# Expert stage of a fused attention, MoE and gated-MLP kernel: half of the middle activations transposed by VectorE from PSUM to PSUM

## What is computed

```python
for e in range(E):                      # E = 8
    for k in range(2):
        mask = top2[:, k] == e
        if not mask.any():
            continue
        h = np.maximum(x[mask] @ w1[e], 0.0)            # 384 -> 1024
        out[mask] += top2_w[mask, k, None] * (h @ w2[e])  # 1024 -> 384
```

## Time and profile before

| | |
|---|---|
| median of three runs | 1359.45 us |
| the profiled execution, own time | 1352.85 us |
| its span, first to last instruction | 1351.1 us |
| mean granted TensorE clock | 0.981 |
| TensorE matmul busy | 1259.0 us, 93% |
| VectorE busy | 613.1 us, 45% |
| ScalarE busy | 463.4 us, 34% |
| GpSimd busy | 444.2 us, 33% |
| expert stage, first `hidden` to last output | 327.4 to 854.9 us |

### The profile page before, as it was taken

How to read it: one execution, slowest core, us unless ns; L and a number is a source line. 1 busy time by engine, 2 the same in 40 slices (tenths; PEclk the granted TensorE clock), 3 DMA queues, 4 the chain that set the end, 5 groups by cost and what they waited for, 6 DMA issues and landing times.

```text
span 1351.1 us, 26279 instructions
## 1 busy us (share of the span) xinstructions
PE 1259.0 (93%) x9117; PEld 1164.4 (86%) x9118; DVE 613.1 (45%) x1150; ACT 463.4 (34%) x975; POOL 444.2 (33%) x375
## 2 busy tenths in 40 slices
PE   4999999993999999999999999299999999999998
PEld 3787878772999999999999999299999999999997
DVE  6888888855222222222222222344444444444433
ACT  3555656642222222222222222232323323232321
POOL 8567787734541505050517600320101101010000
PEclk9999999996999999999999999799999999999999
DMA  8223433115313222222222320220101101010000
GB/s 301 74 93 134 127 128 117 58 62 212 133 48 128 75 100 80 97 90 88 100 78 107 116 105 30 59 59 0 54 18 36 48 6 53 18 35 17 0 18 18
DMA packets 36172, 105.43 MB, mean 78 GB/s; under 512 B 4992, under 2 KB 20352, under 8 KB 33664
## 3 DMA queue, kind: packets, MB, share of 16 engines
q1 hardware_dynamic: 26928, 55.62, 12.3%
q0 software_dynamic: 8592, 47.98, 9.9%
q10 hardware_dynamic: 576, 0.79, 0.2%
HBM read 77.83 MB, written 26.54 MB: 77 GB/s over the span
## 4 chain that ended last, share of the span: by engine, by line
PE 76%; POOL 9%; DVE 5%; ACT 4%; issue 4%; DMA 1%; DVEq 0%; SPq 0%; ACTq 0%; POOLq 0%
PE pD L1504 17%; PE pD L1569 10%; PE pA L1569 10%; PE pS L1528 9%; PE pA L1528 8%; PE pA L1582 6%; PE pA L1320 4%; PE pA L1515 4%; PE pS L1582 3%; PE pX L1486 1%; POOL fT L517 1%; POOL prods L552 1%; POOL qk L536 1%; DVE W L961 1%; POOL qk L535 1%
## 5 line engine op out<-in xcount | busy, mean ns | idle before, releaser
L1504 PE MATMUL pD<-we,xsH 128*128 x660 | 210.0, 400 | 0.8 <-issue 0.8
L686 POOL DMA_INDIRECT pair<-y_sorted,y_row x48 | 49.6, 1034 | 369.1 <-DVE z L1240 277.0
L1320 PE MATMUL pA<-W 64*128 64x128 f32 x1920 | 140.4, 287 | 15.8 <-DVE W L961 12.2
L1320 PEld LDWEIGHTS pA<-W 64*128 64x128 f32 x1920 | 118.6, 190 | 34.4 <-DVE W L961 18.3
L1261 DVE TENSOR_TENSOR gs<-pD,sig 128x384 f32<-128x384 f32 x96 | 53.5, 557 | 195.5 <-ACT sig L897 195.3
L1504 PEld LDWEIGHTS pD<-we,xsH 128*128 128x128 f32 x660 | 120.7, 190 | 23.9 <-issue 1.4
L1504 PE MATMUL pD<-we,xsL 128*128 x330 | 129.8, 393 | 0.0
L640 POOL CAST we<-stage 128x3072 fp32r<-128x3072 f32 x14 | 38.5, 2753 | 251.9 <-PE pS L1528 128.5
L855 ACT CAST hidH<-pA 128x512 fp32r<-128x512 f32 x110 | 59.2, 589 | 173.6 <-PE pA L1515 173.6
L897 ACT ACTIVATE sig<-pD 128x384 f32<-128x384 f32 x96 | 47.3, 492 | 206.9 <-PE pA L1569 206.4
L1528 PE MATMUL pS<-we,hidH 128*128 x448 | 116.5, 341 | 1.8 <-issue 1.8
(11 more groups left out here) (200 smaller groups left out, 2747.4 us busy)
## 6 DMA issues: line engine op xcount, KB each, us to landing
stage<-w POOLq DMA_DIRECT2D x14, 1536.0 KB, 9.2
qk<-qk_t SPq DMA_DIRECT2D x24, 512.0 KB, 3.6
xs<-x_sorted SPq DMA_DIRECT2D x55, 192.0 KB, 2.4
y_sorted<-yo SPq DMA_DIRECT2D x55, 192.0 KB, 1.9
fT<-f_t SPq DMA_DIRECT2D x12, 512.0 KB, 4.2
vN<-v_n SPq DMA_DIRECT2D x24, 256.0 KB, 2.7
out<-fin SPq DMA_DIRECT2D x8, 576.0 KB, 2.8
stage<-w SPq DMA_DIRECT2D x2, 1536.0 KB, 13.6
```

The lines of the kernel that those rows point to most:

```text
L686: pool.indirect_dma_start(out=pair[:, j, k], out_offset=None, in_=y_sorted[:, :], in_offset=bass.IndirectOffsetOnAxis(ap=y_row[:, t * TS + ...
L1320: ins = pe.matmul(pA[par][:, s, c * P:(c + 1) * P], both[r, 1, c], both[r, 0, c], start=True, stop=True)
L1504: ins = pe.matmul(pD[:, h * 512:(h + 1) * 512], (xsL if a else xsH)[t.par][:, k * P:(k + 1) * P], we[:, bass.ds(at + (b * WE + k * F + h * ...
```

## The change

For each tile the middle activations are now treated by halves in two different ways. The first half goes as before: ReLU on ScalarE into `hid`, which now holds 512 values (`HF = F // 2`), then four transposes on TensorE. The second half is not rectified first. VectorE transposes it from its PSUM bank (`hidden_bank(t, 1)`, bank 1 of `pD` for even tiles, bank 1 of `pA[1]` for odd ones) into bank 1 of `pA[0]`, by 16 instructions on 32 partitions, each of four 32x32 blocks. It does eight of them before `low_x` and eight after. A new semaphore, `s_ht`, counts them. `high_h` and `low_h` then apply the ReLU to both halves: `high_h` is an ACTIVATE with Relu, `low_h` a `scalar_tensor_tensor` with max and subtract.

The order changes too: TensorE does `turn_hidden(t+1)` ahead of `output(t)`, and `output` waits for each half of `hidL` on its own. ScalarE does `rectify(t+1)` ahead of `high_x(t+2)`, and it takes over `take_y`, at the end of its slot. In the table, column 0 of `more_than` is set to 1 once at the start, so that an expert without rows has one tile. The diff, without the declarations of `HF`, of the semaphore and of the smaller `hid`:

```diff
@@ -368,6 +370,10 @@
         def y_bank(t):
 
             return pS[:, 0:DM] if t.par == 0 else pA[1][:, 0, 0:DM]
+
+        def hidden_bank(t, h):
+
+            return pA[1][:, 1] if h and t.par else pD[:, h * HF:(h + 1) * HF]
 
         def out_bank(j):
 
@@ -841,30 +847,37 @@
 
             def rectify(t):
                 if t.c >= 1:
-                    act.wait_ge(s_th, t.times(2))
-                for k in range(2):
-                    act.wait_ge(s_g1, t.times(2, k + 1))
-                    act.activation(hid[:, k * 512:(k + 1) * 512], pD[:, k * 512:(k + 1) * 512],
-                                   ACT.Relu).then_inc(s_relu, 1)
-
-            def high_h(t):
+                    act.wait_ge(s_th, t.times(1))
+                act.wait_ge(s_g1, t.times(2, 1))
+                act.activation(hid[:], hidden_bank(t, 0), ACT.Relu).then_inc(s_relu, 1)
+
+            def high_h(t, h):
                 if t.c >= 2:
                     act.wait_ge(s_g2, t.times(1))
-                for k in range(2):
-                    act.wait_ge(s_th, t.times(2, k + 1))
-                    act.copy(hidH[t.par][:, k * 512:(k + 1) * 512], pA[0][:, k]).then_inc(s_hh, 1)
+                act.wait_ge(s_ht if h else s_th, t.times(1, 1))
+                act.activation(hidH[t.par][:, h * HF:(h + 1) * HF], pA[0][:, h], ACT.Relu).then_inc(s_hh, 1)
+
+            def take_y(t):
+                act.wait_ge(s_g2, t.times(1, 2))
+                if t.c >= 2:
+                    act.wait_ge(s_ys[t.par], t.over(2, 16))
+                act.copy(yo[t.par][:], y_bank(t)).then_inc(s_yo, 1)
 
             high_x(Tile(0))
             high_x(Tile(1))
             rectify(Tile(0))
-            high_h(Tile(0))
+            for h in range(2):
+                high_h(Tile(0), h)
 
             def slot(t):
+                if (t + 1).before(SLOTS):
+                    rectify(t + 1)
                 if (t + 2).before(SLOTS):
                     high_x(t + 2)
                 if (t + 1).before(SLOTS):
-                    rectify(t + 1)
-                    high_h(t + 1)
+                    for h in range(2):
+                        high_h(t + 1, h)
+                take_y(t)
             slots(act, slot)
 
 
@@ -1072,8 +1085,8 @@
 
             for t in (*aT, *stateB, hits, zero):
                 dve.memset(t[:], 0.0)
-            for t in (ones, ones_row):
-                ins = dve.memset(t[:], 1.0)
+            for t in (ones[:], ones_row[:], more_than[:, :, 0:1]):
+                ins = dve.memset(t, 1.0)
             ins.then_inc(s_clear, 1)
             dve.wait_ge(s_const, 2)
             dve.tensor_reduce(chunk_sum[:], ident[:].rearrange("p (c e) -> p e c", c=HP)[:, 0:2 * E], AX.X,
@@ -1145,8 +1158,8 @@
             dve.tensor_tensor(count[:], pS[:, 0:E], region_row[:, 0], ALU.subtract)
             step(dve.tensor_tensor(count_i[:], pS[0:1, 0:E], region_row[0:1, 0], ALU.subtract))
 
-            step(dve.tensor_tensor(more_than[:], count[:].unsqueeze(2).to_broadcast([P, E, NT]),
-                                   iota_t[:].unsqueeze(1).to_broadcast([P, E, NT]), ALU.is_gt))
+            step(dve.tensor_tensor(more_than[:, :, 1:], count[:].unsqueeze(2).to_broadcast([P, E, NT - 1]),
+                                   iota_t[:, 1:].unsqueeze(1).to_broadcast([P, E, NT - 1]), ALU.is_gt))
             step(dve.tensor_reduce(tiles_of[:], more_than[:], AX.X, ALU.add))
             step(dve.tensor_tensor_scan(ends[:], ones_row[:], tiles_of[:], 0.0, ALU.mult, ALU.add))
             step(dve.tensor_scalar(last[:], ends[0:1, E - 1:E], -1.0, None, ALU.add))
@@ -1181,18 +1194,23 @@
                 dve.tensor_tensor(xsL[t.par][:], pX[:, 0:DM], xsH[t.par][:].bitcast(F32),
                                   ALU.subtract).then_inc(s_xl, 1)
 
-            def low_h(t):
-                for k in range(2):
-                    dve.wait_ge(s_hh, t.times(2, k + 1))
-                    c = slice(k * 512, (k + 1) * 512)
-                    dve.tensor_tensor(hidL[t.par][:, c], pA[0][:, k], hidH[t.par][:, c].bitcast(F32),
-                                      ALU.subtract).then_inc(s_hl, 1)
-
-            def take_y(t):
-                dve.wait_ge(s_g2, t.times(1, 2))
-                if t.c >= 2:
-                    dve.wait_ge(s_ys[t.par], t.over(2, 16))
-                dve.tensor_copy(yo[t.par][:], y_bank(t)).then_inc(s_yo, 1)
+            def turn_hidden(t, tokens):
+                dve.wait_ge(s_g1, t.times(2, 2))
+                if t.c >= 1:
+                    dve.wait_ge(s_hl, t.times(2))
+                by_32 = [b.rearrange("p (c q a) -> p c q a", q=4, a=32) for b in (hidden_bank(t, 1), pA[0][:, 1])]
+                for i in tokens:
+                    for q in range(4):
+                        ins = dve.transpose(by_32[1][32 * q:32 * (q + 1), :, i], by_32[0][32 * i:32 * (i + 1), :, q])
+                if tokens[-1] == 3:
+                    ins.then_inc(s_ht, 1)
+
+            def low_h(t, h):
+                dve.wait_ge(s_hh, t.times(2, h + 1))
+                c = slice(h * HF, (h + 1) * HF)
+                dve.scalar_tensor_tensor(out=hidL[t.par][:, c], in0=pA[0][:, h], scalar=0.0,
+                                         in1=hidH[t.par][:, c].bitcast(F32), op0=ALU.max,
+                                         op1=ALU.subtract).then_inc(s_hl, 1)
 
             low_x(Tile(0))
             low_x(Tile(1))
@@ -1211,14 +1229,19 @@
                               ALU.add).then_inc(s_yrow, 1)
             dve.wait_ge(s_yrow, 3)
             dve.tensor_tensor(y_row[:], row_of[:], shift[:], ALU.add).then_inc(s_yrow, 1)
-            low_h(Tile(0))
+            turn_hidden(Tile(0), (0, 1, 2, 3))
+            for h in range(2):
+                low_h(Tile(0), h)
 
             def slot(t):
+                if (t + 1).before(SLOTS):
+                    turn_hidden(t + 1, (0, 1))
                 if (t + 2).before(SLOTS):
                     low_x(t + 2)
-                take_y(t)
                 if (t + 1).before(SLOTS):
-                    low_h(t + 1)
+                    turn_hidden(t + 1, (2, 3))
+                    for h in range(2):
+                        low_h(t + 1, h)
             slots(dve, slot)
 
 
@@ -1497,33 +1520,35 @@
                 pe.wait_ge(s_we, ready + 1)
                 pe.wait_ge(s_xl, t.times(1, 1))
                 for h in range(2):
-                    if t.c >= 1:
-                        pe.wait_ge(s_relu, t.times(2, h - 1))
+                    if h == 0 and t.c >= 1:
+                        pe.wait_ge(s_relu, t.times(1))
+                    if h == 1 and t.c >= 2:
+                        pe.wait_ge(s_ht, t.times(1, -1))
                     for k in range(KC):
                         for n, (a, b) in enumerate(PARTS):
-                            ins = pe.matmul(pD[:, h * 512:(h + 1) * 512], (xsL if a else xsH)[t.par][:, k * P:(k + 1) * P],
-                                            we[:, bass.ds(at + (b * WE + k * F + h * 512), 512)],
+                            ins = pe.matmul(hidden_bank(t, h), (xsL if a else xsH)[t.par][:, k * P:(k + 1) * P],
+                                            we[:, bass.ds(at + (b * WE + k * F + h * HF), HF)],
                                             start=k + n == 0, stop=k == KC - 1 and n == 2)
                     ins.then_inc(s_g1, 1)
 
             def turn_hidden(t):
-                for h in range(2):
-                    pe.wait_ge(s_relu, t.times(2, h + 1))
-                    if t.c >= 1:
-                        pe.wait_ge(s_hl, t.times(2, h - 1))
-                    for k in range(4):
-                        ins = pe.transpose(pA[0][:, h, k * P:(k + 1) * P], hid[:, (4 * h + k) * P:(4 * h + k + 1) * P],
-                                           ident[:])
-                    ins.then_inc(s_th, 1)
+                pe.wait_ge(s_relu, t.times(1, 1))
+                if t.c >= 1:
+                    pe.wait_ge(s_hl, t.times(2, -1))
+                for k in range(FC // 2):
+                    c = slice(k * P, (k + 1) * P)
+                    ins = pe.transpose(pA[0][:, 0, c], hid[:, c], ident[:])
+                ins.then_inc(s_th, 1)
 
             def output(t):
 
                 at, ready = weights_of(t)
                 pe.wait_ge(s_we, ready + 2)
-                pe.wait_ge(s_hl, t.times(2, 2))
                 if t.c >= 2:
                     pe.wait_ge(s_yo, t.times(1, -1))
                 for k in range(FC):
+                    if k % (FC // 2) == 0:
+                        pe.wait_ge(s_hl, t.times(2, 1 + k // (FC // 2)))
                     for n, (a, b) in enumerate(PARTS):
                         ins = pe.matmul(y_bank(t), (hidL if a else hidH)[t.par][:, k * P:(k + 1) * P],
                                         we[:, bass.ds(at + ((2 + b) * WE + k * DM), DM)],
@@ -1540,9 +1565,9 @@
                     hidden(t + 1)
                 if (t + 2).before(SLOTS):
                     turn_rows(t + 2)
-                output(t)
```

(5 more changed lines are left out.)

## The result

The changed kernel takes 1337.83 us (median of four runs, 1337.10 to 1340.27), against 1359.59 for the kernel before: 21.8 us less, a ratio of 0.984 with an interval of 0.982 to 0.986. The forecast was 1335.8 against 1359.45, 23.6 us less. Its profiled execution took 1338.19 us with a span of 1336.4.

What follows compares the result with a forecast made beforehand. TensorE, gapless in the expert stage, was taken as the bound. Gains of 22.4 in the slots, 0.5 at the start and 1.2 at the end, less 0.5, gave 23.6 us: 1359.45 to 1335.8, range 1331 to 1344.

Steps and rivals of the forecast that it cites:

- What bounds the kernel: Expert stage's 52 middle slots: TensorE busy without a gap, 9.51 us a slot; VectorE and ScalarE idle some 7 us each.
- Four transposes of eight leave TensorE: Each middle slot: 0.43 us less on TensorE, period 9.08, 22.4 us over 52 slots (20.8 to 22.9).
- Sixteen VectorE instructions come in: Each slot: transposes of about 302 ns at a pitch of 0.30 (0.22 to 0.43), 4.8 us on VectorE, hidden behind TensorE.
- the overlap: VectorE's transposes: consecutive instructions without a wait might overlap, making the pitch 0.22 us, 3.5 us a slot.
- At the start: First two tiles: TensorE idles 1 us behind VectorE's transposes and `rectify(1)`, yet 0.5 us is gained.
- At the end: Last output: covered by `output(53)`, it starts at 849.3 instead of 850.46, 1.2 us gained.
- about 1 us: Sign of being right: TensorE idle this long ahead of tile 1's transposes and as much ahead of the last output.
- `take_y` on ScalarE: After the last output: it delays the `outH` copy by 0.48; 0.5 us lost if the third gather waits for `outL`.
- VectorE as the bound: Rival, middle slots: transposes dearer than 0.43 us set the period; at 0.50 the kernel takes 1395. Chance 0.08.
- the second rival: TensorE's queue: 0.4 us of "issue" ahead of `output` each slot eats the gain, about 1358. Chance 0.04.
- a part of the gain is lost: Rival: waits around `low_x` or the two ReLUs come 0.1 to 0.3 us late a slot, 1346. Chance 0.08.
- The order: `turn_hidden(t+1)` ahead of `output(t)`: no gain in the middle slots; it matters only at the two ends.

Runs made afterwards that it cites:

- both ends on TensorE: Changed kernel, but tiles 0 and 54 transposed wholly on TensorE and the last copy of y on VectorE: 1330.33 us, ratio 0.9824; repeated, 1335.85, 0.9828.
- the same groups: Changed kernel with each VectorE transpose written to the partitions it reads, so the blocks land in the wrong place: 1334.84 us.
- the two later profiles: Changed kernel, unedited, measured twice more: 1333.21 us, ratio 0.9845, and 1340.39 us, ratio 0.986.
- the third pair of medians: Changed kernel, unedited, on another chip: 1340.39 us against 1360.10 for the kernel before, ratio 0.986.
- with 24: Changed kernel with eight more VectorE transposes a slot, copies into a spare SBUF tile: 1395.63 us.
- The run with 20: Changed kernel with four more VectorE transposes a slot, copies into a spare SBUF tile: 1358.12 us against 1360.10 for the kernel before.

## Why the prediction was right, point by point

**What bounds the kernel** held: TensorE without a gap in 52 slots, before and after, and in the runs with the old order, with `take_y` on VectorE, with both ends on TensorE and with the same groups (400.00 of 400 us). Of VectorE's 1.5 us to spare `take_y` used 0.6 without a loss.

**Four transposes of eight leave TensorE**, 0.43 us a slot, 22.4 in all: measured 22.53. The order taken back alone gives the same period, so this is the whole of the gain in the middle.

**Sixteen VectorE instructions come in**: 332 ns where I took 302, and a pitch of 0.34 to 0.35 where I took 0.30, inside the bounds of 0.22 and 0.43. The row of the 192-value copy misled by 30 ns. The rule on quadrants of the Trainium skill, "VectorE: DVE Perf Modes", section "Two Vector instructions with no wait between them", was right against the overlap: with it the pitch is the whole duration; the other half of that choice, 0.22, is what the run with the same groups shows. `low_h` was sized too dear: with a constant for its scalar it takes 692 ns, not 750, against 686 before. The load a slot is 7.5 us with its gaps, where I had 6.9.

**At the start** the mechanism was right and its size was off. I had 0.5 us gained and measured 1.94 lost (2.4 and 3.0 in the two later profiles). Of the 2.4 us between, 16 x 0.045 = 0.7 come from the pitch. The 0.39 of "issue" ahead of the first output I had put at nothing, though I had named it as a rival for every slot. The first output takes 5.80 instead of the 4.45 of one at full clock, 1.4 us more: behind the idle stretch the granted clock fell, which I had not counted. This is the term of the sum that was mis-sized most.

**At the end** I had 1.2 gained and measured 0.4. The pitch takes about 0.6 of the missing 0.8, and the rest is the 0.30 of "issue" ahead of the last output, which I had not counted. The "about 1 us" of TensorE idle that I named as a sign of being right was 1.84 at the start and 1.97 here.

**`take_y` on ScalarE** costs 0.31 to 0.33 ahead of the MLP, where I had 0.5, and the third gather follows `outL` at 0.83 us in all 13.

**The sum**: by the two first profiles, the stage alone changed by -22.53 + 1.94 - 0.39 + 0.31 = -20.7 us, forecast -23.6; the medians say -21.8, -21.9 and -19.7. The rest of the difference between the two first profiles was in parts that the change does not touch. That the first pair of medians came within 2 us of the forecast is in part luck: the stage itself fell short by 2.9 (3.2 at the two ends, 0.3 back elsewhere), and the third pair of medians by 3.9.

**The rivals.** VectorE as the bound did not come about with 16, and does with 24. Its condition I had as 16p + 2.2 above 9.08, that is 0.43 for one. The run with 20 shows the loss begins sooner, by the second rival: a ReLU that ends late uncovers "issue" ahead of `output`. It is not the load alone that decides. 16 at 0.346 leave 1.5 us to spare; four more transposes, 1.3 us ahead of the ones that `high_h` waits for, are too much, while `take_y`, 0.6 us behind everything else, costs nothing. What I called "a part of the gain is lost, 0.1 to 0.3 a slot" is what that run shows, 0.33.

**The order** is where my reasoning had a hole that cost nothing here. I wrote that it brings no gain in the middle and did not ask what it would cost with eight transposes: 117 us.

## What to carry to other kernels

When one engine is busy without a gap and another is half idle, moving work is worth exactly what it took on the first, as long as the second hands on its results early enough: here 8.1 us of work in 9.08 cost nothing with the added piece last, and 8.8 us cost 0.33 a slot with it in front. Count the pitch with every change of partition group. Slow work that is hidden in a loop's middle stands bare at its two ends: keep the first and the last round on the fast engine. And an order of work is right for a given split of it: test the order without the split and the split without the order.

## What the runs showed of the hardware that I had not expected

- TensorE's queue that is held at a wait until shortly before the engine needs its next instruction shows 0.25 to 0.57 us of "issue" ahead of `output` when the wait ended at most 0.24 us before the transposes in between (run with 20), and none when it ended 0.83 us before. `output`'s addresses come from a value read from SBUF; that this read is what takes the time is not shown.
- Idle stretches of about 2 us on TensorE, at the same place of the same loop, left the granted clock at 1.00 in some executions and at 0.50 in others: after 1.97 us ahead of the last output it fell in two of six profiles, which are of four kernels. The output behind took 4.45 us, or 6.0.
- VectorE transposes on 32 partitions, from PSUM to PSUM, that begin at the same partitions as the one ahead follow at 0.20 to 0.25 us; those that write another group follow at 0.33 to 0.36 (0.29 to 0.31 where only every fourth does).
- `scalar_tensor_tensor` with a constant takes 692 ns for 512 values, 6 more than `tensor_tensor`; with a scalar per partition it cost 60 more at 384.
